# The last eight of 48 attention units in another order, with the feed forward's first products among them

## What is computed

```python
a = exp(scores - max); a = a / (sum(a) + 1e-9); x = a @ v        # attention, B=2 H=8 S=768 D=64
x = x.transpose(0, 2, 1, 3).reshape(1536, 512)                   # tokens x model
h = x @ w_in                                                     # 512 -> 2048
P = a0 + a1*h + a2*h*h + a3*h*h*h
Q = 1 + |b0|*|h| + |b1|*h*h
x = (P / (Q + 1e-6)) @ w_out                                     # 2048 -> 512
...                                                              # second feed forward, 512 -> 1024 -> 512
```

## Time and profile before

| what | value |
|---|---|
| median of 3 runs | 481.54 us (480.85 to 481.79) |
| profiled execution, its own time | 480.79 us |
| its span in the profile | 478.9 us |
| PE busy, share of the span | 467.9 us, 98% |
| PEld busy | 382.6 us, 80% |
| DVE busy | 376.2 us, 79% |
| ACT busy | 270.0 us, 56% |
| POOL busy | 60.4 us, 13% |
| granted TensorE clock | 1.00 of full speed |

### The profile page before, as it was taken

One profiled execution on the slowest core, in us unless ns is written; L12 is line 12 of the kernel. 1 busy time (PEld: TensorE's weight loads), 2 busy tenths in 40 slices (PEclk: granted clock), 3 DMA queues, 4 the chain that ended last, 5 costly groups with the idle time before them and its releaser, 6 DMA issues.

```text
span 478.9 us, 7527 instructions
## 1 busy us (share of the span) xinstructions
PE 467.9 (98%) x2734; PEld 382.6 (80%) x2734; DVE 376.2 (79%) x685; ACT 270.0 (56%) x477; POOL 60.4 (13%) x135
## 2 busy tenths in 40 slices
PE   7999989999999999999999999999999999999997
PEld 5667778888888878888887888888888888888885
DVE  6899989999999989778889999999685555555550
ACT  6999998656565555555556445443553333333341
POOL 5989850000000000000000000000000000000000
PEclk9999999999999999999999999999999999999999
DMA  8989864000000000000033445331012222222201
GB/s 294 365 323 335 297 239 179 1 0 1 0 1 0 1 1 0 1 1 1 5 105 89 139 138 170 104 88 44 10 35 67 66 66 66 74 67 76 68 23 44
DMA packets 25665, 42.91 MB, mean 90 GB/s; under 512 B 2080, under 2 KB 16800, under 8 KB 24480
## 3 DMA queue, kind: packets, MB, share of 16 engines
q1 hardware_dynamic: 23760, 36.64, 22.5%
q0 software_dynamic: 1296, 5.24, 3.6%
q10 hardware_dynamic: 576, 0.60, 0.4%
HBM read 33.04 MB, written 3.15 MB: 76 GB/s over the span
## 4 chain that ended last, share of the span: by engine, by line
PE 85%; ACT 8%; DVE 4%; issue 1%; DMA 0%; DVEq 0%; ACTq 0%
PE ps L1220 9%; PE ps L1221 9%; PE ps L1222 9%; PE ps L1152 8%; PE ps L1153 8%; PE ps L1154 8%; ACT probs L499 6%; PE ps L1285 5%; PE ps L1283 5%; PE ps L1284 5%; PE ps L1240 5%; PE ps L1239 5%; PE ps L1238 5%; PE ps L1266 2%; PE ps L1119 1%
## 5 line engine op out<-in xcount | busy, mean ns | idle before, releaser
L1220 PE MATMUL ps<-gate_hi,bank_b_hi 128*128 128x512 f32 x192 | 74.9, 390 | 0.5 <-DVE tok_lo L966 0.5
L1152 PE MATMUL ps<-tok_hi,bank_a_hi 128*128 128x512 f32 x192 | 75.0, 391 | 0.0
L1153 PE MATMUL ps<-tok_lo,bank_a_hi 128*128 128x512 f32 x192 | 74.7, 389 | 0.0
L1222 PE MATMUL ps<-gate_hi,bank_b_lo 128*128 128x512 f32 x192 | 74.7, 389 | 0.0
L1154 PE MATMUL ps<-tok_hi,bank_a_lo 128*128 128x512 f32 x192 | 74.7, 389 | 0.0
L1221 PE MATMUL ps<-gate_lo,bank_b_hi 128*128 128x512 f32 x192 | 74.7, 389 | 0.0
L562 ACT ACTIVATE quad<-ps 128x1024 f32<-128x1024 f32 x23 | 23.7, 1030 | 57.8 <-DVE rest L904 57.8
L499 ACT ACTIVATE probs<-negs,small 128x256 f32<-128x256 f32 (+1 forms) x96 | 45.9, 484 | 1.4 <-DVE small L743 1.1
L459 POOL TENSOR_SCALAR probs<-probs,small 128x256 f32<-128x256 f32 (+1 forms) x96 | 42.6, 467 | 10.7 <-DVE small L754 10.5
L886 DVE SCALAR_TENSOR_TENSOR quad<-quad,small,absh 128x1024 f32<-128x1024 f32 x23 | 29.5, 1282 | 17.9 <-ACT absh L565 17.8
L1220 PEld LDWEIGHTS ps<-gate_hi,bank_b_hi 128*128 128x128 f32 x192 | 36.0, 188 | 8.7 <-issue 1.2
(11 more groups left out here) (107 smaller groups left out, 945.5 us busy)
## 6 DMA issues: line engine op xcount, KB each, us to landing
v_sb<-in_v_win SPq DMA_DIRECT2D x8, 704.0 KB, 6.1
bank_a_raw<-in_w_in SPq DMA_DIRECT2D x4, 1024.0 KB, 8.7
bank_b_raw<-in_w_out SPq DMA_DIRECT2D x4, 1024.0 KB, 7.7
stage_hi<-tok_hi SPq DMA_DIRECT2D x12, 256.0 KB, 2.7
stage_lo<-tok_lo SPq DMA_DIRECT2D x12, 256.0 KB, 2.8
out_dram<-out_sb SPq DMA_DIRECT2D x12, 256.0 KB, 2.0
q_sb<-in_q_t SPq DMA_DIRECT2D x14, 192.0 KB, 4.8
k_sb<-in_k_win SPq DMA_DIRECT2D x7, 384.0 KB, 7.2
```

The source lines that it names most:

```text
L1152: pe.matmul(banks(bank, 1), bank_a_hi[:, f, ws], x_hi, start=(k == 0), stop=False)
L1153: pe.matmul(banks(bank, 1), bank_a_hi[:, f, ws], x_lo, start=False, stop=False)
L1220: pe.matmul(banks(4 + k, 1), bank_b_hi[:, f, ws], g_hi, start=first, stop=False)
L1222: mm = pe.matmul(banks(4 + k, 1), bank_b_lo[:, f, ws], g_hi, start=False, stop=last)
```

## The change

On every engine the last units leave the loop (TAIL = 42) and get a list of their own, `attend_last`. TensorE makes V42/43 before T44/45, and U0 and U1 each stand ahead of a turning: U0, T44/45, U1, T46/47, V44 to V47, U2. Before it was T44/45, V42/43, U0, T46/47, V44 to V47, U1, U2. ScalarE copies 40 ahead of unit 46's exp, writes out 38 and 41 ahead of unit 47's exp, and makes `gate_first_inputs(0)` before copy 46. VectorE makes both pending `attend_low` before the sums of unit 46, has three w_in tiles split before copy 44, three after it and the last two at the very end, and makes `gate_first_poly(0)` right after copy 46. `gate_first_inputs` uses the other `absh` buffer, since probabilities of the last units still stand in the first.

```diff
@@ -248,17 +248,17 @@
     SETUP_STEPS, STEPS_PER_PAIR = 4, 2
     WARM_UP = 7
     LAG = 4
+    TAIL = HEADS - BLOCKS
     GROUPS = FT // 2
     N_GROUPS = CHUNKS * GROUPS
     POOL_IN, SPLITS_AT = 4, (21, 23, 33, 35)
     LOADS_AT, CAST_AT = (1, 3, 4, 5), 7
     LATE_IN = FT - 4
-    IDLE_IN, END_IN = POOL_IN + 5, LATE_IN - 1
+    IDLE_IN = POOL_IN + 5
 
     def outs_at(n):
 
-        return [m for m in range(2, DONE_B0 - 1, 3) if n == m + (3 if m % 2 else 4)] + \
-            [m for m in (DONE_B0 - 1,) if n == HEADS - 4]
+        return [m for m in range(2, DONE_B0 - 3, 3) if n == m + (3 if m % 2 else 4)]
 
     HIGH_ON_DVE = (5, 14, 23, 32)
 
@@ -533,23 +533,39 @@
             for m in outs_at(n):
                 if m not in HIGH_ON_DVE:
                     attend_out(m)
-            if k < HEADS:
-                for h in range(2):
-                    attend_exp(k, h)
+            for h in range(2):
+                attend_exp(k, h)
             attend_copy(n)
-            if n == HEADS - 4:
-                for j in range(POOL_IN // 2, LATE_IN // 2):
-                    split_in_high(j)
-            if k < HEADS:
-                for h in range(2):
-                    attend_exp(k + 1, h)
+            for h in range(2):
+                attend_exp(k + 1, h)
+
+        def attend_last():
+
+            attend_copy(TAIL - 2)
+            for h in range(2):
+                attend_exp(HEADS - 2, h)
+            attend_out(TAIL - 4)
+            attend_copy(TAIL)
+            attend_out(TAIL - 1)
+            for h in range(2):
+                attend_exp(HEADS - 1, h)
+            for j in range(POOL_IN // 2, LATE_IN // 2 - 1):
+                split_in_high(j)
+            attend_copy(HEADS - 4)
+            gate_first_inputs(0)
+            split_in_high(LATE_IN // 2 - 1)
+            attend_copy(HEADS - 2)
+            attend_out(HEADS - 4)
+            gate_first_inputs(1)
+            attend_out(HEADS - 1)
+            split_out_high(0)
 
         def gate_first_inputs(f):
 
             src, cs = banks(f, 1), slice(f * CH, (f + 1) * CH)
             act.wait_ge(hidden_ready, f + 1)
             act.activation(quad[:, cs], src, ACT.Square).then_inc(first_in, 1)
-            act.activation(absh[0][:, cs], src, ACT.Abs, scale=coef_b[:, 0:1]).then_inc(first_in, 1)
+            act.activation(absh[1][:, cs], src, ACT.Abs, scale=coef_b[:, 0:1]).then_inc(first_in, 1)
             act.activation(poly[:, cs], src, ACT.Identity, scale=coef_a[:, 3:4],
                            bias=coef_a[:, 2:3]).then_inc(first_in, 1)
 
@@ -587,13 +603,9 @@
                     attend_exp(n, h)
             act.wait_ge(coefs_loaded, 16)
             act.activation(abs_b1, coef_b[:, 1:2], ACT.Abs).then_inc(act_const, 1)
-            for n in range(0, HEADS, 2):
+            for n in range(0, TAIL - 2, 2):
                 attend_pair(n)
-            attend_out(HEADS - 4)
-            gate_first_inputs(0)
-            attend_out(HEADS - 1)
-            split_out_high(0)
-            gate_first_inputs(1)
+            attend_last()
         with act.Else():
             act.wait_ge(coefs_loaded, 16)
             act.activation(abs_b1, coef_b[:, 1:2], ACT.Abs).then_inc(act_const, 1)
@@ -791,33 +803,45 @@
 
             k = n + AHEAD
             pr, m = divmod(k, NPB)
-            if k < HEADS:
-                if pr and m == 0:
-                    dve.wait_ge(pool_bias, 4 * pr - 2)
-                attend_shift(k, 0)
-            if k < HEADS:
-                attend_shift(k, 1)
-            if n == HEADS - 4:
-                attend_low(DONE_B0 - 1)
+            if pr and m == 0:
+                dve.wait_ge(pool_bias, 4 * pr - 2)
+            attend_shift(k, 0)
+            attend_shift(k, 1)
             attend_copy(n)
-            if n == HEADS - 4:
-                for f in range(POOL_IN, IDLE_IN):
-                    split_in_low(f)
-            if n + SUMS_AHEAD < HEADS:
-                attend_sums(n + SUMS_AHEAD)
-            if k < HEADS:
-                if pr and m == 0:
-                    dve.wait_ge(pool_bias, 4 * pr)
-                attend_shift(k + 1, 0)
-            if n + SUMS_AHEAD < HEADS:
-                attend_reciprocals(n + SUMS_AHEAD)
-            if k < HEADS:
-                attend_shift(k + 1, 1)
-            if n != HEADS - 4:
-                for m_out in outs_at(n):
-                    if m_out in HIGH_ON_DVE:
-                        attend_high(m_out)
-                    attend_low(m_out)
+            attend_sums(n + SUMS_AHEAD)
+            if pr and m == 0:
+                dve.wait_ge(pool_bias, 4 * pr)
+            attend_shift(k + 1, 0)
+            attend_reciprocals(n + SUMS_AHEAD)
+            attend_shift(k + 1, 1)
+            for m_out in outs_at(n):
+                if m_out in HIGH_ON_DVE:
+                    attend_high(m_out)
+                attend_low(m_out)
+
+        def attend_last():
+
+            attend_copy(TAIL)
+            attend_low(TAIL - 4)
+            attend_low(TAIL - 1)
+            attend_sums(HEADS - 2)
+            attend_reciprocals(HEADS - 2)
+            for f in range(POOL_IN, IDLE_IN - 2):
+                split_in_low(f)
+            attend_copy(HEADS - 4)
+            for f in range(IDLE_IN - 2, IDLE_IN + 1):
+                split_in_low(f)
+            attend_copy(HEADS - 2)
+            dve.wait_ge(coefs_loaded, 16)
+            dve.wait_ge(act_const, 1)
+            gate_first_poly(0)
+            attend_low(HEADS - 4)
+            attend_low(HEADS - 1)
+            gate_first_poly(1)
+            split_out_low(0)
+            for f in range(IDLE_IN + 1, LATE_IN):
+                split_in_low(f)
+
         def full_attention():
 
             dve.wait_ge(f_index, 2)
@@ -870,7 +894,7 @@
 
             src, cs = banks(f, 1), slice(f * CH, (f + 1) * CH)
             dve.wait_ge(first_in, 3 * f + 2)
-            dve.scalar_tensor_tensor(quad[:, cs], quad[:, cs], abs_b1, absh[0][:, cs], ALU.mult,
+            dve.scalar_tensor_tensor(quad[:, cs], quad[:, cs], abs_b1, absh[1][:, cs], ALU.mult,
                                      ALU.add).then_inc(quad_ready, 1)
             dve.wait_ge(first_in, 3 * f + 3)
             dve.tensor_tensor(poly[:, cs], poly[:, cs], src, ALU.mult).then_inc(poly_ready, 1)
@@ -934,19 +958,9 @@
                 attend_shift(n, 1)
                 if n % 2:
                     attend_reciprocals(n - 3)
-            for n in range(0, HEADS, 2):
+            for n in range(0, TAIL, 2):
                 attend_pair(n)
-            attend_low(HEADS - 4)
-            dve.wait_ge(coefs_loaded, 16)
-            dve.wait_ge(act_const, 1)
-            for f in range(IDLE_IN, END_IN):
-                split_in_low(f)
-            gate_first_poly(0)
-            attend_low(HEADS - 1)
-            split_out_low(0)
-            gate_first_poly(1)
-            for f in range(END_IN, LATE_IN):
-                split_in_low(f)
+            attend_last()
         with dve.Else():
             full_attention()
             for f in range(POOL_IN, LATE_IN):
@@ -1124,6 +1138,8 @@
 
             for m in (n, n + 1):
                 attend_turn(m)
+            if n >= TAIL:
+                return
             for m in (n + SCORES_AHEAD, n + SCORES_AHEAD + 1):
                 if m < HEADS:
                     attend_scores(m)
@@ -1160,15 +1176,17 @@
         with pe.If(take == 1):
             for n in range(FIRST_SCORES, SCORES_AHEAD):
                 attend_scores(n)
-            for n in range(0, HEADS, 2):
+            for n in range(0, TAIL + 2, 2):
                 attend_two(n)
-                if n == HEADS - 4:
-                    pe.wait_ge(shifted_ready, 2 * HEADS)
-                    up(0)
-            for n in (HEADS - 2, HEADS - 1):
+            for n in range(TAIL - 2, TAIL + 2):
                 attend_values(n)
             pe.wait_ge(shifted_ready, 2 * HEADS)
+            up(0)
+            attend_two(HEADS - 4)
             up(1)
+            attend_two(HEADS - 2)
+            for n in range(HEADS - 4, HEADS):
+                attend_values(n)
             up(2)
         with pe.Else():
             pe.wait_ge(shifted_ready, 2)
```

## The result

The changed kernel takes 482.02 us in the median of 22 runs, the kernel before 480.90 us in the median of 22: ratio 1.0022, 95% interval 1.0015 to 1.0030. It is slower by 1.1 us, where 0.95 was forecast; the time itself was forecast as 482.5 us. The span of the profiled execution went from 478.9 to 480.0 us.

The account below looks back on a forecast made before the run. TensorE, then VectorE's unbroken pile up to up(8), was taken to bound the stretch; `gate_quotient(0)` 0.95 us later passes to up(8): 481.54 + 0.95 = 482.5 us. Own range 482.1 to 482.9, whole range 481.0 to 483.4.

Parts of the forecast that it names:

- What bounds: TensorE limits up to about 76 us, then VectorE's unbroken work from 81.63 to 104.08; the start of `gate_quotient(0)` decides.
- Copy 40 first: ScalarE's copy 40 ahead of two exps lets T42/43 start at about 64.29 instead of 64.95, 0.66 us earlier.
- U0: U0 waits for `attend_low(41)` and starts at 67.21 against 68.13; TensorE is really ahead by 0.27 us.
- Turnings between ups: U0 to the next turning takes 2.95 us; U2 starts at 76.57 against 76.74, so TensorE gains 0.17 us.
- VectorE: VectorE idles 1.2 us until copy 46 at 74.53; 8.05 us follow, so `gate_quotient(0)` starts at 82.58, 0.95 us later.
- The wait for out 47: `attend_low(47)` on VectorE waits for ScalarE's out 47 until 77.7, ready at 77.64: 0.1 us more.
- The hidden collision: GpSimd's scaling of units 46 and 47 now runs beside VectorE's splits; costed at nothing, VectorE's idle time taking it.
- Rival 3: Scaling and splits slow each other down at double cost, copy 46 at 75.8: +2.2 us, 483.7; chance 0.08.
- The other terms costed at nothing: The other `absh` buffer and SP's last two, later w_out loads, with over 15 us of cover: no cost.
- Rival 2: VectorE doesn't hold up(8), reaches `gate_quotient(0)` by 81.63, or the wait is only the profile's model: 0.55 us won, 481.0; chance 0.12.
- Rival 4: TensorE wins all its idle time in the stretch, 1.26 us: 480.3; chance 0.08.

Follow-up runs that it names:

- e1: Changed kernel with the last two low splits of w_in moved from the list's end into VectorE's idle time ahead of copy 46; 480.81 us, ratio 1.0000.
- e2: Changed kernel with the splits of w_in's tiles 12 to 15 moved from groups 0 and 1 to groups 2 and 3, behind up(8); 481.13 us, ratio 1.0007.
- e5: Changed kernel with VectorE's gap ahead of copy 46 filled by two splits and w_in's last four splits moved behind up(8); 480.51 us, ratio 0.9992.
- e4: Kernel before with only the change's early order on ScalarE and VectorE, up to the sums of unit 46; 482.01 us, ratio 1.0010.
- e6: As e4 on the kernel before, but unit 47's exps stand ahead of out 41 and the sums ahead of low 41; 480.55 us, ratio 0.9984.
- e8: Changed kernel with the first three low splits behind copy 44 instead of ahead of it; 482.42 us, ratio 1.0032.
- e3: Kernel before with the splits of w_in's last four tiles moved to groups 2 and 3, behind up(8); 480.48 us, ratio 0.9984.
- e7: As e6 on the kernel before, with the splits of w_in's last four tiles moved behind up(8) as well; 480.09 us, ratio 0.9983.

## Why the prediction was right, point by point

- **What bounds.** Right, and shown by e1, e2 and e5: with TensorE's order of the change untouched, taking 1.2 to 3.6 us out of VectorE's pile moved up(8) by 0.93 to 1.66 us, and with VectorE out of the way the changed order is a small gain. From `gate_quotient(0)` to up(8) I took 22.45 us; the changed kernel has 105.12 - 82.67 = 22.45, and the four other kernels whose up(8) waits (e1, e4, e6, e8) 22.46 or 22.47, while `gate_quotient(0)` itself ranges from 18.92 (e6) to 20.84 us (e8) from T40/41.
- **Copy 40 first.** Forecast 0.66 us for T42/43. From T40/41 it started 1.97 us later instead of 2.58: 0.61.
- **U0.** Forecast 4.84 us from T40/41 (67.21 - 62.37), measured 4.98. V42/43 did wait for low 38, and U0 for low 41, and U0 started 0.15 us after low 41's end (67.03), not 0.05: the hand-over was sized too small.
- **Turnings between ups.** Each U and turning came in 2.91 and 2.96 us where I took 2.95. V44 to V47 took 1.98 instead of 2.16, so U2 gained 0.25, not 0.17.
- **VectorE.** Copy 46 was forecast at 12.16 and was at 12.26 after an idle time of 1.12 us (forecast 1.2). From there to `gate_quotient(0)` I added up 8.05 and it took 8.21: low 47 started 0.71 us after low 44 and not 0.57, since it waits for ScalarE's out 47. The wait for out 47 was foreseen, at 0.1 us; it cost 0.24 (0.71 against the 0.47 of low 44 in the earlier trace rows). These are the two terms that were sized too small: 0.10, which comes from U0's hand-over, and 0.16, together the 0.26 between the forecast 0.95 and the 1.21 at up(8).
- **The hidden collision.** I costed the scaling beside the splits at nothing, because VectorE's idle time would take it. So it did in the changed kernel: VectorE lost 0.2 us ahead of copy 44, for which it then waited 0.41 all the same. But e4 shows that it isn't nothing in general. Rival 3 had GpSimd's side nearly right (3.30, where doubled cost is 3.67) and VectorE's wrong (2.10 against 1.88 for three splits), so copy 46 wasn't late. Its own sum doesn't come out either: three splits of 1.2 us from 68.5 end at 72.1, not 73.4, and after copy 44 and three more splits copy 46 would stand at 74.5, no later than in the forecast. The rule of the Trainium skill (SBUF — State Buffer, Who interferes with whom) is borne out in its kind: scaling 3.30 us beside splits, 1.84 without them in e8. Whether either is shut out for a whole instruction, no run here takes apart.
- **The other terms costed at nothing.** The `quad` rows with the other `absh` buffer take 0.74 us (before 0.74 and 0.75), and no split of w_out on ScalarE waits for its load.
- **The rivals.** Rival 2 needed `gate_quotient(0)` by 81.63: it came at 82.67. Its other form, that the wait is only the profile's model, falls with e3, where up(8) came earlier by 0.35 us when VectorE's work was taken away. Rival 4 would have needed the wait at up(8) to go; it grew from 0.38 to 0.45.
- **How near it was.** The difference is what was forecast well: 0.95 against 1.12 us of the medians and 1.21 at up(8), inside the forecast's own +0.6 to +1.4. The time was not: 482.02 lies under the forecast's own 482.1 to 482.9 and only inside the whole range, because the sum stood on a median of 3 executions (481.54) and the 22 have 480.90. The forecast stood on the line of 0.2%, and the result stands just above it. That it was slower at all is shown by the interval; that it was more than 0.2% slower isn't, since the interval begins at 0.15%.

## What to carry to other kernels

When the busiest engine is made to wait less, look for the next engine's unbroken pile of work and ask when it can begin: here a turning moved behind one more up cost VectorE a 1.1 us hole that nothing filled, and the pile behind it passed that on to TensorE in full. Work without a near deadline, such as the splits of weights that are read only three or four groups later, belongs behind the pile's last due time or into the hole; either is worth more here (0.93 and 1.14 us at up(8) of the changed kernel) than the new order itself (0.1, e5 against e3), and the fastest kernel, e7, keeps TensorE's old one. And if GpSimd has work on a chain of waits, keep it apart in time from VectorE instructions like the splits, with two inputs in SBUF, since here both paid for the overlap.

## What the runs showed of the hardware that I had not expected

Who pays for GpSimd and VectorE running side by side isn't fixed: in the changed kernel four scalings went from 1.84 to 3.30 us and three splits from 1.88 to 2.10; in e4 the scalings took 2.79 and five splits 3.57 instead of 3.10. And the start of T40/41, with nothing edited ahead of it, varied by 1.7 us between the profiled executions (62.16 in e7, 63.86 in e8), more than the whole effect of the change; without a mark inside the kernel to measure from, single executions would have misled. The traces show where it arises, within the first 15 us: the turning of units 2 and 3 on TensorE starts at 13.06 us in e7 and at 14.72 in e8, and ahead of it the eight matmuls of the scores with 256 columns that come first (6.46 and 7.04 us) take 1.13 us in e7 and 2.08 in e8. Their weight loads take 0.73 us in the seven executions with an early T40/41 and 1.35 or 1.36 in the three with a late one (e2, e4, e8). The granted clock reads 1.00 in both stretches, and why the same matmuls took longer stays open.
